# The matrix engine's branch moved ahead of the first expert chunk, and that chunk's input in two column parts

## What is computed

```python
# x: 3072 x 384, from the attention stage
logits = xn @ en.T / tau
expert_idx = np.argmax(logits, axis=1)
gate_w = probs[np.arange(N), expert_idx]
for e in range(8):
    mask = expert_idx == e
    h = np.maximum(x[mask] @ w1[e], 0.0)          # w1: 384 x 1024
    out[mask] = gate_w[mask, None] * (h @ w2[e])  # w2: 1024 x 384
# then, over all tokens: max of three products with 384 x 768, and a product with 768 x 384
```

## Time and profile before

| | us |
|---|---|
| median of 3 runs | 738.59 (738.5 to 741.81) |
| the profiled execution, its own time | 744.38 |
| its span | 742.7 |
| PE busy in it | 704.6 (95%) |
| DVE busy | 303.6 (41%) |
| ACT busy | 274.2 (37%) |
| POOL busy | 348.4 (47%) |
| PE's share of the chain that ended last | 78% |
| mean granted clock of PE | 0.979 |

### The profile page before, as it was taken

The page is one execution under the profiler, slowest core; times in us unless marked ns, Lnnn a source line. Parts: engine busy times, 40 slices in busy tenths (PEclk is TensorE's granted clock), DMA queues, the critical chain, the costliest instruction groups (busy, mean ns, idle before and its releaser), DMA issues.

```text
span 742.7 us, 13379 instructions
## 1 busy us (share of the span) xinstructions
PE 704.6 (95%) x5274; PEld 621.5 (84%) x5275; DVE 303.6 (41%) x649; ACT 274.2 (37%) x588; POOL 348.4 (47%) x275
## 2 busy tenths in 40 slices
PE   5899899968989999999999999999999999999995
PEld 4798788855979999999999978888888888888884
DVE  7899698977111221212212163422323223223221
ACT  4889798872424344343443121111111111111100
POOL 5135344565656587775877919242250430420112
PEclk9999999987989999999999999999999999999998
DMA  9999876114452863724453134002002000000001
GB/s 192 204 211 189 217 155 163 66 69 158 156 173 85 277 207 108 241 86 158 152 162 87 50 105 146 1 21 93 12 26 78 21 21 0 22 21 1 21 22 42
DMA packets 131156, 78.32 MB, mean 105 GB/s; under 512 B 106088, under 2 KB 121200, under 8 KB 131088
## 3 DMA queue, kind: packets, MB, share of 16 engines
q1 hardware_dynamic: 121840, 61.08, 30.2%
q0 software_dynamic: 4320, 10.72, 4.3%
q10 hardware_dynamic: 4928, 5.62, 2.3%
HBM read 62.63 MB, written 14.77 MB: 104 GB/s over the span
## 4 chain that ended last, share of the span: by engine, by line
PE 78%; issue 12%; DVE 3%; POOL 2%; ACT 0%; POOLq 0%; ACTq 0%; DVEq 0%
PE bank L1595 44%; PE bank L1622 5%; PE bank L1623 5%; PE bank L1624 5%; PE bank L1368 4%; PE bank L1465 3%; PE bank L1406 3%; PE bank L1474 2%; PE bank L1572 2%; PE bank L1416 2%; PE bank L1453 1%; POOL out L637 1%; PE bank L1395 1%; PE bank L1359 1%; DVE lg L1036 0%
## 5 line engine op out<-in xcount | busy, mean ns | idle before, releaser
L1595 PE MATMUL bank<-yh,mh 128*128 128x512 f32 x324 | 126.9, 392 | 1.2 <-ACT tm L917 1.2
L1595 PE MATMUL bank<-yh,ml 128*128 128x512 f32 x324 | 127.5, 394 | 0.0
L578 POOL TENSOR_TENSOR wsp<-raw,wsp 128x1536 fp32r<-128x1536 f32 x28 | 97.9, 3508 | 39.5 <-ACT wsp L877 39.4
L637 POOL DMA_INDIRECT out<-oo,ids x24 | 23.7, 988 | 197.1 <-DVE oo L1308 197.1
L1277 DVE SCALAR_TENSOR_TENSOR hTl<-bank,hTh 128x432 fp32r<-128x432 f32 x64 | 38.9, 608 | 187.9 <-ACT hTh L859 154.6
L1595 PE MATMUL bank<-xh,wsp 128*128 128x432 f32 x384 | 90.1, 371 | 3.5 <-issue 3.0
L1595 PE MATMUL bank<-yl,mh 128*128 128x512 f32 x324 | 91.7, 391 | 0.0
L859 ACT ACTIVATE hTh<-bank 128x432 fp32r<-128x432 f32 x64 | 34.0, 531 | 124.3 <-PE bank L1595 98.0
L1595 PEld LDWEIGHTS bank<-xh,wsp 128*128 128x128 f32 x384 | 72.5, 192 | 8.4 <-issue 3.3
L920 ACT CAST gh<-t 128x512 fp32r<-128x512 f32 x36 | 22.3, 621 | 151.8 <-DVE t L1319 151.8
L1595 PEld LDWEIGHTS bank<-yh,mh 128*128 128x128 f32 x324 | 60.9, 188 | 14.0 <-ACT tm L917 1.6
(11 more groups left out here) (238 smaller groups left out, 1249.5 us busy)
## 6 DMA issues: line engine op xcount, KB each, us to landing
raw<-in_moe_w SPq DMA_DIRECT2D x14, 1536.0 KB
expert_columns<-ye ACTq DMA_DIRECT2D x8, 648.0 KB
nat<-in_k SPq DMA_DIRECT2D x32, 144.0 KB, 3.0
nat<-in_q SPq DMA_DIRECT2D x32, 144.0 KB, 3.9
vt<-in_v SPq DMA_DIRECT2D x32, 144.0 KB, 3.0
attention_rows<-xc SPq DMA_DIRECT2D x4, 1152.0 KB, 6.7
yT_ff<-expert_columns SPq DMA_DIRECT2D x6, 768.0 KB
nat<-in_alpha SPq DMA_DIRECT2D x30, 144.0 KB, 4.0
```

The source lines that it names most:

```text
L578: g.tensor_tensor(wsp[:, to, 1, n, part], raw[:, n, part], wsp[:, to, 0, n, part].bitcast(f32), ALU.subtract).then_inc(w_lo[n], 1)
L637: g.indirect_dma_start(out=out, out_offset=bass.IndirectOffsetOnAxis(ap=ids[:, i, 0:1], axis=0), in_=oo[i % 2][:], in_offset=None).then_in ...
L1595: last = mm(o, x, y, start=(n == 0), stop=(n == len(todo) - 1))
```

## The change

- PE: the wait for `r_tab` at 1 and the branch on `many_t` stand ahead of `lift_first` and chunk 0, and both bodies now begin with these. The `Else` body has two more calls of `keep_warm` ahead of `lift_first`.
- `lift_first`: the transposed input lies in four banks. Columns 0 to 255 (the first two gathered tiles) go to banks 6 (two feature groups side by side) and 7, columns 256 to 431 to banks 4 and 5. The first part is announced by `p_xa` behind the second tile. The filler behind the last tile is gone, and the filler writes to bank 3.
- ACT and DVE split the first part first (`a_xa`, `d_xa`), then the second.
- `first_up`: up(0), up(1), up(2) of chunk 0 run over the first 256 columns, then over the other 176: 54 matmuls instead of 27, with the same arithmetic. The blocks count as done behind the second part.
- DVE: the chunk tables up to `cont_t` come first and release `r_tab` at 1; then the gate block; `chunk_rows`, `chunk_counts`, `positions` and the gate's sum come behind `h_low` of blocks 2, 3, 4 and 5. `r_tab` is counted up to 4; POOL's `fetch(1)` and ACT's store wait for 2, the records for 4.
- Some small tables get another place in SBUF, as they now live beside the weights being loaded.

```diff
@@ gpsimd @@
-        pool.wait_ge(r_tab, 1)
+        pool.wait_ge(r_tab, 2)
...
         pool.wait_ge(r_gate, 1)
-        pool.wait_ge(r_tab, 2)
+        pool.wait_ge(r_tab, 4)
@@ build @@
+    xb = lambda b, n, w: bank[b][:, 0:n * w].rearrange("p (k n) -> p k n", k=n)
+    first_a = ((xb(6, 2, XA), slice(0, 2), slice(0, XA)), (xb(7, 1, XA), slice(2, 3), slice(0, XA)))
+    first_b = ((xb(4, 2, CW - XA), slice(0, 2), slice(XA, CW)), (xb(5, 1, CW - XA), slice(2, 3), slice(XA, CW)))
@@ scalar @@
-        for k in range(KD):
-            x_high(0, k)
+        act.wait_ge(p_xa, 1)
+        for turned, ks, cs in first_a:
+            a.copy(xh[:, ks, cs], turned).then_inc(a_xa, 1)
+        act.wait_ge(p_xt, KD)
+        for turned, ks, cs in first_b:
+            a.copy(xh[:, ks, cs], turned).then_inc(a_xh, ks.stop - ks.start)
@@ vector @@
-        chunk_rows()
-        chunk_counts()
-        for k in range(KD):
-            x_low(0, k)
+        for n, (turned, ks, cs) in enumerate(first_a):
+            dve.wait_ge(a_xa, n + 1)
+            d.tensor_tensor(xl[:, ks, cs], turned, xh[:, ks, cs].bitcast(f32), ALU.subtract).then_inc(d_xa, 1)
...
-        chunk(0, 0, positions)
+        chunk(0, 0, (chunk_rows, chunk_counts, positions, make_gates))
@@ tensor @@
                 for k in range(KD):
-                    last = tr(bank[(6, 7, 3)[k]][:, P * j:P * j + n], xg[j][0:n, P * k:P * k + P], ident[0:n, 0:n])
-                    if j == len(RT) - 1:
-                        last.then_inc(p_xt, 1)
-                keep_warm(1, bank[4])
+                    (part, _k, _c), at = (first_a, first_b)[j // 2][k // 2], P * (j % 2)
+                    last = tr(part[:, k % 2, at:at + n], xg[j][0:n, P * k:P * k + P], ident[0:n, 0:n])
+                if j % 2:
+                    last.then_inc((p_xa, p_xt)[j // 2], (1, KD)[j // 2])
+                if j < len(RT) - 1:
+                    keep_warm(1, bank[3])
...
+            def first_up():
+                pe.wait_ge(w_lo[0], CR)
+                for part, cs, high, low in ((0, slice(0, XA), (a_xa, 2), (d_xa, 2)),
+                                            (1, slice(XA, CW), (a_xh, KD), (d_xl, KD))):
+                    pe.wait_ge(*high)
+                    for f in range(3):
+                        last = three(bank[f][:, cs], [(w1_of(0, k, f), w1_of(1, k, f), xh[:, k, cs], xl[:, k, cs])
+                                                      for k in range(KD)], [low], moving_last=True)
+                        if part:
+                            last.then_inc(p_h, 1)
...
         keep_warm(WARM_X, bank[3])
-        lift_first()
-        chunk(0, 0, 0)
         pe.wait_ge(r_tab, 1)
         with many_chunks(pe):
+            lift_first()
+            chunk(0, 0, 0)
             chunks_left(pe, 0, 0, 0, chunk)
...
         with pe.Else():
-            for e in range(1, E):
+            keep_warm(2, bank[3])
+            lift_first()
+            for e in range(E):
                 chunk(e, e % 2, e)
```

More of the change, by code:

```diff
@@ L233, in build @@
     assert cur[0] <= ff_low
+    cur[0] = attention_end
+    chunk_f, base_f = sb("chunk_f", [P, MC + 1]), sb("base_f", [P, 1])
+    tcmp = sb("tcmp", [P, MC + 1, E])
+    tcmps = sb("tcmps", [P, MC + 1, E])
+    tsum = sb("tsum", [P, 6, MC + 1])
+    sh = sb("sh", [P, NT, E])
+    rv = {n: sb("v_" + n, [P, NT]) for n in ("r", "sqr", "s", "sc", "sum")}
+    assert cur[0] <= (top - 3584) // 512 * 512
     router_const = (top - 3584) // 512 * 512
@@ L886, in chunk @@
             if isinstance(i, int) and i == 0:
-                act.wait_ge(r_tab, 1)
+                act.wait_ge(r_tab, 2)
             y_out_of(i)
@@ L1199, in x_low @@
         def x_low(i, k):
-            b = ((6, 7, 3) if isinstance(i, int) and i == 0 else (6, 7, 6))[k]
+            b = (6, 7, 6)[k]
             dve.wait_ge(a_xh, KD * i + k + 1)
             d.tensor_tensor(xl[:, k, :], bank[b][:, 0:CW], xh[:, k, :].bitcast(f32), ALU.subtract).then_inc(d_xl, 1)
[L1204 to L1208, removed]
         NE, NC = E - 1, MC + 1
@@ L1226, in _ @@
         d.tensor_tensor(cont_t[:], rw["nc"][:].rearrange("p (e o) -> p e o", o=1).to_broadcast([P, E, E]),
[L1227 to L1232, removed]
+                        iot[:, 0:E].rearrange("p (o c) -> p o c", o=1).to_broadcast([P, E, E]), ALU.is_gt
+                        ).then_inc(r_tab, 1)
+        link(d.tensor_tensor(sh[:], lg[:], over(mx24[:], NT), ALU.subtract))
+        dve.wait_ge(r_sqrt, 1)
+        exact_norm(root[:], ss[:], rv["s"][:], rv["r"][:], rv["sqr"][:])
+        link(d.reciprocal(rv["sc"][:], rv["s"][:]))
+        d.tensor_tensor(sh[:], sh[:], over(rv["sc"][:], NT), ALU.mult).then_inc(r_sh, 1)
         def chunk_rows():
@@ L1278, in h_low, with chunk @@
                                    ALU.max, ALU.subtract).then_inc(d_h, 1)
-        def chunk(i, par, between=None):
+        def chunk(i, par, between=()):
             for f in range(KF):
                 h_low(i, f)
-                if f == 0 and between is not None:
-                    between()
+                if f - 2 in range(len(between)):
+                    between[f - 2]()
             for k in range(KD):
                 x_low(i + 1, k)
-        chunk(0, 0, positions)
+        chunk(0, 0, (chunk_rows, chunk_counts, positions, make_gates))
         with few_chunks(dve):
@@ L1625, in down @@
                 last.then_inc(p_d, 1)
-            up(0)
-            up(1)
+            def first_up():
[8 more added lines that the diff above has]
+                            last.then_inc(p_h, 1)
+            if isinstance(i, int) and i == 0:
+                first_up()
+            else:
+                up(0)
+                up(1)
             for f in range(2, KF):
-                up(f)
+                if f > 2 or not (isinstance(i, int) and i == 0):
+                    up(f)
                 down(f - 2)
```

25 lines of the change are left out of this document (14 added, 11 removed).

## The result

The changed kernel takes 746.78 us (median of 16 runs, 742.89 to 751.83) against 738.55 (16 runs, 736.44 to 744.58) on the same chip: a ratio of 1.0105, with a 95% interval from 1.0082 to 1.0128. It is slower by some 8 us, where 1.8 less was forecast. Its profiled execution took 746.0 us.

The account below looks back on a forecast made before the run. The matrix engine was taken to bound the kernel, through idle time or slow clock; -5.7 + 1.6 + 0.6 + 1.7 = -1.8 us took the median from 738.59 to 736.8 us, range 734.0 to 740.6.

Parts of the forecast that it names:

- 5, the tables between feature blocks: VectorE's tables behind blocks 2, 3 and 4 of chunk 0: longest 2.0 us, hidden; chunk 1's fetch has 0.7 to spare.
- the unforeseen: Anywhere in the kernel: outcomes that neither the forecast nor any listed alternative covers, chance 0.05.
- Step 6: Gates last and memory moved: nobody waits for the gate before POOL's records near 220, so it costs nothing.
- Step 1, the boundary: End of chunk 0: removing the branch saves the 2.99 us pause and 2.72 us of slow clock, 5.7 us.
- Steps 2 and 3: Chunk 0's front: early jump of 3.63 us, then warm-ups and transposes on the path; first product 1.6 us later.
- step 3: Behind the jump: two more warm-up calls (1.3 us) and transposes, first product at 182.4 instead of 180.84, +1.6 us.
- the clock's term: Matrix engine's 1.8 us pause at the early jump: the clock is taken to fall, costing 1.7 us.
- the clock stays up: Rival at the early jump: the clock doesn't fall over the short pause; sum -3.5 us, 735.1 us, chance 0.22.
- a second fetch: Rival behind the early jump: the next instruction page waits behind weight loads; +5.9 us, sum +4.1, 742.7 us, chance 0.08.
- the jump didn't wait for the queued matmuls: Denies a rival at the early branch: jump begins only at 176.1, after queued matmuls; sum +1.8, 740.4 us, chance 0.04.
- Step 4, the narrow products: Chunk 0's first three blocks in two column parts: spacings 0.12 and 0.10, 5.9 us in all, +0.6 us.
- The step of 5.8 us: Whole kernel: the median lies 5.8 us below before's profiled execution, carried over unchanged, turning 742.6 into 736.8.

Follow-up runs that it names:

- the trials: Changed kernel plus, behind its whole work, twelve and in another run sixteen small VectorE instructions beside four back-to-back GpSimd subtractions; the run of twelve took 912.96 us in all.
- the twelve later trials: Of sixteen instructions appended to the changed kernel, varying arrival and GpSimd's next wait, the twelve not starting with GpSimd's run; they lasted 1.45 to 13.05 us.
- the third experiment: Kernel before with the positions table behind block 3 of chunk 0 in place of block 0: 739.25 us, ratio 1.0003.
- the second experiment: Changed kernel with GpSimd waiting for the positions before its four low-part subtractions for expert 1 instead of behind them: 739.9 us, ratio 1.0008.
- eight warm-ups: Against the changed kernel with positions computed early: eight warm-up calls ahead of the branch in place of four, none behind it; 743.65 us, ratio 1.0056.
- first experiment: Changed kernel with VectorE computing record positions ahead of the first input part instead of behind block 4 of chunk 0: 745.67 us, ratio 1.0085.

## Why the prediction was wrong

**The step that failed is 5, the tables between feature blocks.** It priced the tables by the longest, 2.0 us, from rows in which GpSimd at most issued gathers, and found all of it hidden, with 0.7 us to spare for the fetch. The fetch was indeed in time (no pause ahead of chunk 1's transposes). But it named GpSimd's four low splits only as something queued behind the table, and never asked what the tables' instructions do beside them. One of them was held for 13.82 us, 6.9 of which show: 5.1 as a pause, the rest in matmuls at the lower clock. Moving the run of GpSimd alone brings the ratio from 1.0105 to 1.0008, and the trials show the hold behind the kernel's own work. None of the prediction's five rivals names it; it belongs to the 0.05 for the unforeseen. Step 6 fails with it: "nobody waits for the gate" is true of its result, but its tensor_scalar stands in VectorE's queue ahead of hTl, and cost nearly as much as the addition had when that was out of the way (1.0085 against 1.0105).

The trace of before had a trace of it, which I didn't read. Its 36 subtractions gl of VectorE, in one form, with min, median and max:

```profile
L1321 DVE TENSOR_TENSOR gl<-t,gh x36: 692/693/2532, 442.0 to 718.5; 128x512 fp32r<-128x512 f32 x36
```

The one at 2532 ns started at 466.40, while GpSimd subtracted from 465.70 to 468.38. A maximum of 3.7 times the median in a form that does the same thing each time was a question to ask; its 1.8 us would have put a price on the rival that was missing.

The Trainium skill, SBUF — State Buffer, section Who interferes with whom, says that VectorE and GpSimd share a pair of SBUF ports as an exclusive lock: a VectorE instruction with two SBUF inputs is blocked by a GpSimd instruction that reads SBUF, as are copies and tensor_scalars in two-port modes, while a reduction, or an instruction with at most one SBUF input outside these modes, is not. On who is held, the nine forms of the trials agree with it. That page of the Trainium skill says that the lock is held for the whole instruction, here 3.4 us; seven of the twelve later trials and three kernels show 11 to 14 us across four GpSimd instructions, and there the measurement decides. Had the addition been held for one GpSimd instruction, it would have cost at most 3.5 us; in the third experiment 3.01 us were hidden.

**Step 1, the boundary, was right.** 5.9 us gained by the two profiled executions (5.7 predicted); no idle time, clock 1.00, ACT's read hidden. In the third experiment, which has before's boundary, it cost 10.81 instead of 11.41 (50.37 - 39.56), so what goes away is 5.3 to 5.9.

**Steps 2 and 3, the jump and the front, were too small by 0.6.** The first product came 3.86 us later than before, relative to inv_i; step 3 and the clock's term had 1.6 + 1.7 = 3.3. The jump started as early as predicted (2.78 us after inv_i, 2.98 expected) but took 4.41 us instead of 3.63. The matrix engine paused 2.82 us instead of 1.8, half of the difference by the longer jump and half because the warm-ups ahead of it ended earlier (4.4 us after inv_i instead of 5.0): their clock had risen earlier, as the prediction had thought possible. The warm-ups behind the jump ran at half clock: the four from 174.13 to 176.85 took 2.7 us, twice the 1.3 of step 3.

The clock's paragraph reasoned as if the clock were at 1.00 when the pause begins. By its own row it was 0.50 up to 176. In the changed kernel's execution it had risen before the pause and fell within it. In the second experiment's profiled execution it was 0.50 over the warm-ups (to 176.7), 0.81 over 176.7 to 177.5, with the engine idle, and 1.00 from there, and the four warm-ups behind the pause of 2.02 us took 1.56 us. So the outcome of the rival *the clock stays up* came (first product at 11.75), but by a clock that rose within the pause and not by one that stayed.

Two other rivals did not come. Behind the jump nothing waited for a second fetch: the changed kernel's weight loads began at 174.41, right behind the jump's end at 174.1, and from there to the first product down its timeline shows no pause. And the jump didn't wait for the queued matmuls.

**Step 4, the narrow products:** 6.31 us for the 54 instead of 5.43 for 27 wide ones, from first product to first product down: +0.9, where +0.6 was taken. The spacing was 0.12 for 256 columns as predicted and 0.11 for 176, where 0.10 was taken.

**The sum without the hold.** The second experiment is the changed kernel without the long hold: 1.0008 [0.9994, 1.0023], which is -0.4 to +1.7 us, against the -1.8 of the prediction. So even without the missing step the forecast was 1.4 us or more too good. Four sizes add up to 2.0, each an estimate from single executions: the front (0.6), the narrow products (0.3), the boundary (5.3 instead of 5.7: 0.4), and before's own front, which was 0.7 dearer in its profiled execution than in the third experiment's. The step of 5.8 us from before's profiled execution to its median was carried over unchanged, and that was wrong for the kernel after: its profiled execution (746.0) lies 0.8 below its median. The time at which inv_i ended alone differed by 4.2 us between the two profiled executions and by 6.4 us among those of this study; where it lay in the median execution no trace shows.

## What to carry to other kernels

Before small VectorE instructions are put "between" others, look at what GpSimd computes at that time, and at their form: with both inputs in SBUF, or as copy or tensor_scalar out of SBUF, an instruction of 0.2 us can last as long as GpSimd's whole run of back-to-back work, and everything queued behind it on VectorE waits too. An input in PSUM, a place well ahead of the run, or a wait that starts the run behind the instruction costs nothing. In a trace of before, compare maximum and median of each form, and when a wait on a jump can't be avoided, queue enough matmuls ahead of it to last through the jump.

## What the runs showed of the hardware

- **A held VectorE instruction is let in at the first boundary of GpSimd's run or at its end.** Of the 25 holds read here beside three or four back-to-back subtractions (8 and 12 in the trials, five in the kernels), 15 ended with the first and 10 with the last, none between. Which of the two isn't explained.
- **A jump of the matrix engine cost between 3.3 and 6.4 us** in these kernels. The earlier branch took 3632 ns before and 3309 to 3766 in the other runs; the branch on many_t took 4410 in the changed kernel, 3.85 to 4.48 in the experiments that have it early, and 5915 before and 6.37 in the third experiment, where it stands under the weight loads. That the loads make it dear isn't shown: the two places differ in more than that.
- **The clock after a pause:** with 1.00 before the pause, it was 1.00 behind pauses of 0.94 us (eight warm-ups) and 1.16 (before), and 0.50 behind 2.63 (first experiment) and 2.82 (the changed kernel), as behind 2.99 before. Behind before's 2.54 it was still 0.91 over the first microsecond of work and 0.50 after that. With 0.50 before it, a pause of 2.02 us ended at 1.00 (second experiment).
- **Narrow matmuls:** 256 columns follow one another every 0.123 us and 176 columns every 0.110, where 432 columns took 0.197. From 256 to 176 columns, 31% fewer, the spacing fell by 11% only.
